# Loading and splitting the first pass's weights one round later, behind the value tiles

## The reference

```python
out_up = np.repeat(sm_attn(q_d, k_d, v_d), 4, axis=2)
mask = np.abs(pos[:, None] - pos[None, :]) < 4
x = out_up + softmax(where(mask, scale * q @ k.T, -1e9)) @ v
x = (silu(x @ w_gate) * (x @ w_val)) @ w_out        # 512 -> 1536 -> 512
x = relu(x @ w2_in) ** 2 @ w2_out                   # 512 -> 2048 -> 512
```

## Time and profile before

| | us |
|---|---|
| median of 3 runs (lowest, highest) | 924.17 (920.74, 924.63) |
| the profiled execution's own time | 926.48 |
| its span, first to last instruction | 924.7 |
| TensorE busy (98% of the span) | 909.2 |
| VectorE busy (70%) | 650.9 |
| ScalarE busy (43%) | 400.4 |
| GpSimd busy (24%) | 219.8 |

### The profile page before, as it was taken

The page is one execution under the profiler, slowest core; times in us unless marked ns, Lnnn a source line. Parts: engine busy times, 40 slices in busy tenths (PEclk is TensorE's granted clock), DMA queues, the critical chain, the costliest instruction groups (busy, mean ns, idle before and its releaser), DMA issues.

```text
span 924.7 us, 17274 instructions
## 1 busy us (share of the span) xinstructions
PE 909.2 (98%) x6762; PEld 879.0 (95%) x6762; DVE 650.9 (70%) x1112; ACT 400.4 (43%) x733; POOL 219.8 (24%) x278
## 2 busy tenths in 40 slices
PE   8899999999999999999999999999999999999998
PEld 5698999999999999999999999999999999999998
DVE  7685756564576757796757799585879575778775
ACT  3474555554446343455343445242535242525331
POOL 5784545452262000422000223000313000202000
PEclk9899999999999999999999999999999999999999
DMA  9953333231242020421311230010332020221422
GB/s 219 220 175 105 105 103 97 72 99 32 87 126 68 2 69 1 123 83 35 103 35 69 74 133 1 1 35 1 103 103 69 0 70 1 80 80 35 137 69 69
DMA packets 70881, 71.38 MB, mean 77 GB/s; under 512 B 27280, under 2 KB 58000, under 8 KB 70800
## 3 DMA queue, kind: packets, MB, share of 16 engines
q1 hardware_dynamic: 68496, 65.55, 24.3%
q10 hardware_dynamic: 2304, 4.72, 1.5%
HBM read 56.10 MB, written 14.16 MB: 76 GB/s over the span
## 4 chain that ended last, share of the span: by engine, by line
PE 85%; DVE 6%; ACT 3%; DMA 2%; issue 2%; POOL 1%; SPq 1%; ACTq 0%; DVEq 0%; POOLq 0%
PE mlp_ps L975 13%; PE mlp_ps L977 12%; PE mlp_ps L976 12%; PE sc L975 5%; PE sc L977 5%; PE sc L976 5%; PE xp L977 4%; PE xp L975 4%; PE xp L976 4%; PE sd L975 3%; PE sd L977 2%; PE sd L976 2%; PE tr L975 2%; PE tr L977 2%; PE tr L976 2%
## 5 line engine op out<-in xcount | busy, mean ns | idle before, releaser
L1388 ACT ACTIVATE wh_hi<-hbuf 128x384 fp32r<-128x384 f32 x144 | 70.8, 522 | 79.5 <-DVE hbuf L1674 57.1
L694 POOL TENSOR_TENSOR w_raw<-w_raw 128x256 f32<-128x256 f32 x16 | 14.3, 894 | 355.4 <-DMA w_raw<-w_in 355.4
L1682 DVE TENSOR_TENSOR wh_lo<-hbuf,wh_hi 128x384 fp32r<-128x384 f32 x144 | 76.5, 560 | 24.5 <-ACT wh_hi L1388 21.0
L1637 DVE TENSOR_TENSOR ring<-ring_raw,ring 128x768 fp32r<-128x768 f32 x96 | 90.9, 969 | 0.0
L1337 ACT ACTIVATE ring<-ring_raw 128x768 fp32r<-128x768 f32 x96 | 75.3, 836 | 28.8 <-DVE ring_raw L1631 28.5
L975 PE MATMUL mlp_ps<-ring,w_hi 128*128 128x384 f32 x240 | 80.3, 334 | 0.4 <-ACT snap L1368 0.4
L977 PE MATMUL mlp_ps<-ring,w_lo 128*128 128x384 f32 x240 | 80.2, 334 | 0.0
L976 PE MATMUL mlp_ps<-ring,w_hi 128*128 128x384 f32 x240 | 80.2, 334 | 0.0
L975 PE MATMUL mlp_ps<-wh_hi,w_hi 128*128 128x384 f32 x216 | 73.0, 338 | 2.3 <-DVE wh_lo L1682 1.2
L976 PE MATMUL mlp_ps<-wh_lo,w_hi 128*128 128x384 f32 x216 | 72.2, 334 | 0.0
L977 PE MATMUL mlp_ps<-wh_hi,w_lo 128*128 128x384 f32 x216 | 72.2, 334 | 0.0
(11 more groups left out here) (208 smaller groups left out, 2671.7 us busy)
## 6 DMA issues: line engine op xcount, KB each, us to landing
ring_raw<-x_whole SPq DMA_DIRECT2D x24, 384.0 KB, 3.7
ring_raw<-y_whole SPq DMA_DIRECT2D x24, 384.0 KB, 3.7
qk_sb<-qT SPq DMA_DIRECT2D x16, 288.0 KB, 3.3
qk_sb<-kT SPq DMA_DIRECT2D x16, 288.0 KB, 4.2
v_grp<-v SPq DMA_DIRECT2D x32, 144.0 KB
x_whole<-x_f ACTq DMA_DIRECT2D x16, 288.0 KB, 2.3
y_whole<-ypart SPq DMA_DIRECT2D x3, 1536.0 KB, 6.3
v_win<-v SPq DMA_DIRECT2D x64, 64.0 KB, 2.8
```

The lines of the kernel that those rows point to most:

```text
L694: nc.gpsimd.tensor_tensor(block(5), block(7), block(4), ALU.add).then_inc(s_usum[i], 1)
L1388: nc.scalar.activation(hi[:, f, t, :], hbuf[:, e, :], ACT.Copy).then_inc(s_shhi, 1)
L1637: nc.vector.tensor_tensor(ring[:, SLOTS[g][p], 1, :, :], whole(g, p), ring[:, SLOTS[g][p], 0, :, :].bitcast(F32), ALU.subtract).then_inc(s ...
L1682: nc.vector.tensor_tensor(lo[:, f, t, :], hbuf[:, e, :], hi[:, f, t, :].bitcast(F32), ALU.subtract)\
```

## The change

In words:

- Loads: units 0, 1, 2 are loaded in rounds 1, 2, 3 (were 0, 1, 2), units 3 and 4 in round 4, units 5 and 6 in slot 0, unit 7 in slot 1. Inside a round they are issued after the value groups, not first. In rounds 3 and 4 q and k of a later pair are issued after the weights.
- Rounding on ScalarE: unit 0 at the end of round 3 and unit 1 at the end of round 4 (were near the start of rounds 1 and 2); unit 2 in slot 0, and so on one slot later each, units 6 and 7 in slot 4.
- Remainders: unit 0's is still GpSimd's, now last in round 3 (was in round 1). Unit 1's goes from GpSimd (round 3) to VectorE in slot 0, unit 2's to slot 1, and so on, units 6 and 7 in slot 5. In a slot VectorE makes them ahead of the gate product.

```diff
-ROUND_LOAD = {0: [0], 1: [1], 2: [2], 3: [3], 4: [4, 5]}
-SLOT_LOAD = {0: [6, 7]}
-ROUND_HI = {1: [0], 2: [1], 3: [2]}
-SLOT_HI = {0: [3], 1: [4], 2: [5], 3: [6], 4: [7]}
-SLOT_LO_ON_DVE = {0: [2], 1: [3], 2: [4], 3: [5], 4: [6, 7]}
+ROUND_LOAD = {1: [0], 2: [1], 3: [2], 4: [3, 4]}
+SLOT_LOAD = {0: [5, 6], 1: [7]}
+ROUND_HI = {3: [0], 4: [1]}
+SLOT_HI = {0: [2], 1: [3], 2: [4], 3: [5], 4: [6, 7]}
+SLOT_LO_ON_DVE = {0: [1], 1: [2], 2: [3], 3: [4], 4: [5], 5: [6, 7]}
@@ sp_round
-            for i in ROUND_LOAD.get(n, []):
-                load_unit(sp, i)
-            load_qk(sp, n + 3)
+            if n < PAIRS - 1:
+                load_qk(sp, n + 3)
             load_windows(sp, n + 1)
             if n < PAIRS:
                 load_groups(sp, n + 1)
+            for i in ROUND_LOAD.get(n, []):
+                load_unit(sp, i)
+            if n >= PAIRS - 1:
+
+                load_qk(sp, n + 3)
@@ pool_round
-                if n == 1:
-                    first_weight_lo(g, nc.gpsimd, 0)
                 downsample_v(g, n)
                 if n == PAIRS - 1:
-                    first_weight_lo(g, nc.gpsimd, 1)
+                    first_weight_lo(g, nc.gpsimd, 0)
@@ act_round
-            for i in ROUND_HI.get(n, []):
-                act_weight(a, i)
...
             if last:
                 act_split_x(a, n - 1)
                 act_exp_ds(a, n)
-                return
-            act_move_loc1(a, n)
-            act_exp_ds(a, n)
-            act_move_loc2(a, n)
+            else:
+                act_move_loc1(a, n)
+                act_exp_ds(a, n)
+                act_move_loc2(a, n)
+            for i in ROUND_HI.get(n, []):
+                act_weight(a, i)
@@ dve_slot
-            dve_mlp(d, *mlp_at(g), 1)
             for i in SLOT_LO_ON_DVE.get(g, []):
                 first_weight_lo(d, nc.vector, i)
+            dve_mlp(d, *mlp_at(g), 1)
             dve_mlp(d, *mlp_at(g), 2)
```

## The result

The changed kernel takes 935.26 us (median of 6 runs, 933.17 to 936.65). The kernel before, run beside it, takes 920.70 (6 runs, 920.02 to 924.63). The ratio is 1.0142, 95% interval 1.0124 to 1.0161, so it is slower by 11 to 15 us (14.6 by the two medians). Forecast were 932.2 us, 8.0 more than before. The front's median of 924.17 rests on three runs; with three more it is 920.70.

The account below looks back on a forecast made before the run. TensorE was taken as the bound from the slots on. At full clock -6.0 + 3.2 + 4.0 + 1.2 + 1.4 = +3.8, plus clock losses 2.5 + 1.7, gave +8.0 on 924.17: 932.2 us, range 924.5 to 937.

Parts of the forecast that it names:

- the four new waits: TensorE waits for weight remainders in round 4 and ahead of slots 1, 2 and 4: +3.2, +4.0, +1.2, +1.4 us.
- the first fall of the clock: TensorE's work after round 4's wait runs at the lower clock, stretched by 1.75: +2.5 us.
- the gain in rounds 1 to 3: Both TensorE stalls in rounds 2 and 3 and the slow clock stretch go: -6.0 us; least gain 3.2, most 7.
- second fall: Lower clock after slot 1's wait stretches the work ahead of ScalarE's copies in slot 1: +1.7 us.
- the rival with late values of pair 3: Values land as late as before (40.8), round 4 waits 7.9 us instead of 3.2: 936.9 us; chance 0.11.
- the rival with one fall of the clock: Clock holds at one of two gaps: sum +5.5 or +6.3 us; chance 0.25 for holding at one or both.
- Round 4, +3.2: TensorE's first use of unit 0 waits for ScalarE's rounding and GpSimd's remainder: +3.2 us (2.7 to 5).
- Slot 1, +4.0: TensorE waits at slot 1's start for unit 1's remainder from VectorE: +4.0 us (3.1 with a 1.22 us remainder).
- Slots 2 and 4, +1.2 and +1.4: TensorE waits for VectorE's remainders of units 2 and 4: +1.2 us (2.1 with 2.11) and +1.4 us (0 to 1.8).
- Loads, 0: Later weight, q and k loads cost 0 us; unit 3 up to 3 us if transfers took 8 us each.
- VectorE did not get ahead: Rival: VectorE advances during TensorE's round 4 wait, later waits shrink or vanish: -2.0 us, 922.2 us; chance of faster 0.09.
- The terms did not cancel: Rival: 6.0 us gain offsets cheaper remainders, unit 4's hidden, clock holds: +1.0 us, 925.2 us; chance 0.15.

Follow-up runs that it names:

- the second trace: Kernel before, no edit, traced again: 922.4 us (12 runs), ratio 1.0004 to 1.0030.
- unit 0 early: Changed kernel with unit 0 rounded early in round 3 and its remainder made by GpSimd ahead of that round's value sum: 929.4 us, ratio 1.0090.
- slots as before: Changed kernel with remainders of units 2 to 7 in the kernel before's slots and behind the gate product: 932.2 us, ratio 1.0119.
- unit 1 early: Changed kernel with unit 1 rounded at round 3's end, its remainder made by VectorE in round 4 ahead of pair 3's branch sum: 932.7 us, ratio 1.0117.
- the filled gap: Changed kernel with 25 more filler matmuls on TensorE ahead of the first gate tile in round 4: 933.5 us, ratio 1.0125.
- The changed kernel with more to transfer: Changed kernel with the loads of units 0 and 1 issued twice, 1.05 MB more: 936.6 us (4 runs), ratio 1.0130 to 1.0187.
- loads as before: Changed kernel with all loads issued in the order and rounds of the kernel before: 934.0 us (6 runs), ratio 1.0134.
- the first attempt: Changed kernel's late loads; units 0 to 2 rounded early, units 3 to 7 rounded and remaindered as in the kernel before: 925.4 us, ratio 1.0039.
- only the order on VectorE: Kernel before with VectorE making the remainders ahead of the gate product in the slots: 924.0 us (12 runs), ratio 1.0030.
- before, more to transfer: Kernel before with the loads of units 1 and 2 issued twice, 1.05 MB more: 924.4 us (10 runs), ratio 1.0030.

## Why the prediction was right, and where it was not

**The direction was right, and so were the four new waits and the first fall of the clock. The term that failed is the gain in rounds 1 to 3, "-6.0".** Against the execution that I read it came out (36.17 against the forecast 36.57). But it was read from one execution with late transfers and carried over to the median, of which it is no part. The front's own numbers held a warning: that execution lay 2.3 us above the median and 5.7 above the fastest run (920.74), as much as the whole gain.

The terms against the two traces of the kernel before, by the milestones (the first matmul of slot 0 stands at 47.35 in the front's trace, 41.53 in the second and 46.63 in the trace after; in the second trace it waits 1.00 us for GpSimd's split of x, which the other two do not):

| up to | forecast | against the front's trace | against the second |
|---|---|---|---|
| round 4 | -6.0 | -6.3 | 0.0 |
| first gate matmul | +3.2 | +4.0 | +4.0 |
| slot 0 (first fall of the clock) | +2.5 | +1.7 | +0.6 |
| slot 1 | +4.0 | +4.4 | +4.4 |
| slot 2 (second fall 1.7, wait 1.2) | +2.9 | +1.2 | +1.2 |
| slot 4 | +1.4 | +1.8 | +1.8 |
| sum | +8.0 | +6.8 | +12.0 |

The medians differ by 14.6. Of that, 2.1 is the distance of the changed kernel's profiled execution from its own median. Its other five runs have mean clocks of 0.991 to 0.994 against 0.995, so more time at the lower level is likely in most of them; no trace of one was taken.

**What was luck.** The 935.3 us lie near the upper end of the range, 937, which is where the rival with late values of pair 3 stood (936.9), and they did not come late. No rival put the gain in the rounds at nothing; even the least gain was 3.2. In the two executions that the traces compare, the rival with one fall of the clock (+6.3) is closer to the +6.8 than the forecast is.

**Round 4, +3.2:** TensorE came 4.0 us later to the gate tile, 3.72 of it idle. As forecast it was GpSimd's queue (38.83, forecast 38.4), not the rounding. The value groups landed at 36.6, forecast 36.1. With unit 0 early the wait is gone. Other kernels with the same rounds came 3.1 ("slots as before") and 4.1 us ("unit 1 early") later.

**Slot 1, +4.0:** 4.4 us from slot 0 to slot 1, of which 2.8 are slot 0 at the lower clock and 1.64 the wait. That what slot 0 loses lies inside this wait was forecast so. Where slot 0 runs at full clock the wait is 4.19. The remainder took 2.48 us beside GpSimd, not 2.11. It took 1.22 us where GpSimd was idle (60.06 in the trace after), 2.48 where GpSimd was summing the value groups. The rule of the Trainium skill on the shared port pair ("SBUF — State Buffer", section "SBUF: two separate sides") agrees in kind.

**Slots 2 and 4, +1.2 and +1.4:** 0.99 and 1.56 us, unit 2's remainder at 1.22 as taken. Taking both away won 3 us.

**The clock, +2.5 and +1.7.** The first fall came. It cost 1.7 us up to slot 0's first matmul (5.4 us from the gate tile in the trace after, 3.7 in the front's). One part of the difference is that the clock fell 1.0 us after the gap, and I had stretched the whole of it; I had also put that work at 3.3 us where it is 3.72 - 0.50 = 3.2. (The row at 47.35 is slot 0's first matmul, not the last value product; the times are nearly the same.) The second fall did not come, because the first had slowed slot 0 so far that only 1.64 us of gap were left. I had added both as if they were independent. Unit 0 early and the filled gap show the second fall when the first is taken away. The changed kernel with more to transfer shows both, when the first is over ahead of slot 0. Gaps of 2.29, 3.72, 4.19 and 4.86 us had 0.50 in or behind them; the wait that was filled did not, and neither did gaps of 0.94 and 1.64 us. The Trainium skill's rule ("TensorE: Matmul & The Clock Gate", section "What's actually happening"), that activity releases the throttle, agrees with the gap that was filled.

**Loads, 0:** right for the changed kernel, as "loads as before" shows. The estimate of up to 3 us for a late unit 3 was the risk that the first attempt ran into, 4.68 us on ScalarE.

**The rivals.** VectorE did not get ahead (it idled 6.83 us for the held value products). The late transfers did not take the gap's place (the values of pair 3 landed at 36.6). The terms did not cancel: the new waits and the first fall came in full.

## What to carry to other kernels

Ahead of summing terms from one profiled execution, set its time against the spread of the runs: a stall that is as large as the distance between them may be that execution's own, above all one that ends on a transfer while the DMA engines are full. When a preparation step is moved later, look for the first instruction of the bound engine that needs it and follow each engine's own queue back from there; a place "at the end of the round" can be ahead of that use by nothing. Waits and clock losses in a row are not added up, since each changes the size of the next.

## What the runs showed of the hardware that I had not expected

- The same program moved 218 and 266 GB/s in the same 16 us stretch with the DMA engines at 1.02 and 0.93 busy share; what makes the difference stays open.
- After the gap of 3.72 us the granted clock fell 1.0 us *after* TensorE had begun again (gate tile at 41.23, lower level from 42.2), and stayed low for 10.2 us although TensorE was busy for 9.70 of them. With the stall of 2.29 us it fell at about 35.7, just ahead of the work (35.83), and was low for 6.8 us (the windows of the earlier trace rows show 6.4 of them); with the gap of 4.19 us it fell 1.2 us ahead of the work and was low for 6.8; behind the gap of 2.21 us in "only the order on VectorE" it was low for 3.4.
- The length of a gap alone did not decide it. 1.92 us (before, more to transfer) and 2.21 us had the lower clock behind them; 2.02 us (first attempt) and 2.68 us (slot 1 in "slots as before") did not. What does decide stays open.
- A 128x1024 subtraction on VectorE took 1.22 us with GpSimd idle, and beside GpSimd 1.85 (first attempt), 2.11 (the front's trace) and 2.48 us (after).
